# One gate product for both token halves in 32 stationary columns, in a kernel of attention and two expert layers

## The chip, the cores and the metric
One Trainium2 chip, one NeuronCore. The metric is the device time of one execution in microseconds (us), from the runs' own clock; beside it one execution was profiled, and its span runs from its first to its last instruction. Engines: TensorE (PE; its weight loads are PEld), VectorE (DVE), ScalarE (ACT), GpSimd (POOL) and SyncE (SP).

## The reference
Three layers, one behind the other: clustered attention (16 heads of 768 tokens, 64 wide), a routed expert layer (each of 1536 tokens goes to one of 8 experts) and a dense expert layer, in which the change lies. The last one is:

```python
def _moe2_ref(x, w_gate, w1, w2):          # x 1536x512, w_gate 512x8, w1 8x512x1024, w2 8x1024x512
    logits = x @ w_gate
    logits = logits - logits.max()
    P = np.exp(logits)
    for _ in range(8):
        P /= P.sum(1, keepdims=True) + 1e-09
        P /= P.sum(0, keepdims=True) + 1e-09
        P *= N / E
    out = np.zeros((N, D))
    for e in range(E):
        h = np.maximum(x @ w1[e], 0.0)
        out += P[:, e:e + 1] * (h @ w2[e])
    return out
```

## The kernel before
The program runs through attention (to about 310 us), the routed layer (19 tiles of 128 gathered tokens, to about 580 us), and the dense layer (to the end). Each engine has its own instruction list, written by hand, and semaphores join them; there is no planner. An engine works through its list in order, so a wait stops all that stands behind it.

**Numbers in two parts.** Products are made in fp32r with each operand split into a high part (a copy, `split_hi`, L877 to 879, ScalarE) and a low part (the operand less the high part, `split_lo`, L882 to 884, VectorE); a product of two operands is three: high x high, high x low, low x high. The profile gives the helper's line, L879 or L884, for all of them.

**The dense layer** splits tokens in halves (768 each, rows 1 and 2 of a 2x2 scheme), and the inner dimension in halves as well, and forms 7 products of sums of quarters where 8 would be plain ones. `XH[chunk]` and `XL[chunk]` hold, for one of two chunks of 384 tokens of each half (GN = 384), the transposed tokens' high and low parts as seven combinations, each of 2 slices of 128 rows: B11 (first half's tokens, first 256 inputs), B21 (first half's, last 256), B22 (second half's, last 256), T1 (second half's first 256 less first half's), and T2 to T4. The second half's first 256 inputs are so B11 + T1. A unit (L1369 on TensorE, L1635 on ScalarE, L2027 on VectorE) makes one 128-wide slice of two hidden halves for one chunk: seven `multiply` groups of 6 matmuls with 384 moving columns (L1321, L1323, L1324), and among them the six `second` groups of the unit before (L1344 to L1346, 6 matmuls with 512 moving columns each), whose sums VectorE adds to the output (L1959, L1962, L1968). Each expert has 8 units, so there are 64. Units alternate between the PSUM banks `ps_a[0]`, `ps_b[0]` and `ps_a[1]`, `ps_b[1]`; gate work of unit 1 uses the free ones of the other parity.

**The gate logits** are made in unit 1 of the first expert. `WG` (512x8 weights, 128 partitions x 4 x 8) is split in the last routed tile, by ScalarE (L1563) and VectorE (L1919), into `WGS` [128, 4, 16]: the high part in columns 0 to 7, the low part in 8 to 15 of each of 4 slices. `gate_logits(g, turn)` (L1287) makes a product with 16 stationary columns and 384 tokens moving into `ps_a[0]`, for g = 0 to 3: g % 2 is the chunk and g // 2 the token half. For the first half it takes B11 and B21 (4 slices), for the second B11, T1 and B22 (6 slices), each times the high and the low tokens (L1299). ScalarE copies the result to `LT` in SBUF (`read_logits_t`, L1604, L1608). `fold_logits` (L1303) then takes three 128-column pieces of `LT` as the stationary operand, with the small matrix `fold_e` (16x8, two identities on top of each other) moving (L1309), which transposes the logits to tokens on partitions and adds the high and low halves, into `ps_l` (bank `ps_b[0]`). Four turns follow each other: the next product waits until ScalarE has read the one before (`logits_t_out`), and ScalarE waits for the fold of the one before (`logits`). In the order of TensorE in unit 1: S2 stands for the `multiply` group of that name, and so on.

A11, S1, A12, second 0, gate(0), S2, fold(0), gate(2), second 1 and 2, S3, fold(2), gate(1), second 3 and 4, A22, fold(1), gate(3), second 5, S4, fold(3); then unit 2: A11, wait for `max_found`, S1.

VectorE copies the folded logits to `PROB` (L2081) at the end of its unit 1, behind the sum L2077 and the low part L1949 (which itself waits for ScalarE's relu L1676), and finds the maximum (L2083). Unit 2 of TensorE waits for that copy (L1388) ahead of its group S1, which overwrites the bank.

**The last routed tile** (L1913 on VectorE, L1559 on ScalarE, L1253 on TensorE) already sums token halves (`token_sums`: VectorE L1829 and L1831, GpSimd L2156 and L2159) and transposes and splits them for the dense layer (TensorE L1238; ScalarE `hi_parts`, VectorE `lo_parts`). On VectorE: `token_sums` 0 and 1, the gate's low part, the low part of the routed second weights, and the first `lo_parts`. On GpSimd ahead of the routed tiles (L2188 to L2200): two gathers (L2124), a memset of a zero tile (L2196), and the tile-row products (L2200). The constants, `fold_e` among them, are made by GpSimd at the very start (L94 to L117).

Of the kernel before, what the change touches and what calls it, by code (L numbers as in the profile page):

```python
# [72 lines left out]
def constants(nc, mem):  # L73
# [4 lines left out]
        "fold_e": mem.sbuf("fold_e", [2 * E, E]),  # L78
# [12 lines left out]
IDENT, ALL_MADE = 5, 9 + H - 1  # L91


def build_constants(pool, c, made):  # L94
# [20 lines left out]
    pool.wait_ge(made, 9)  # L115
# [757 lines left out]
GROUPS = NT // GT  # L873
# [31 lines left out]
def expert_layers(nc, sems, attn, c, X, L, w1, w2, xs, out_row, w_gate, dense_w1, dense_w2, out_dram, W1R, W1H, W1L,  # L905
                  w1_at, stationary_at, scratch_at, w1_loaded, x_stored):

    with ExitStack() as stack:
# [67 lines left out]
        WGS = mem.sbuf("w_gate_hi_lo", [P, DC, 2 * E], F32R)  # L976
# [31 lines left out]
        LT = mem.at("logits_t", [2 * E, GN], F32, stationary_at + 2 * STATIONARY * 4)  # L1008
# [26 lines left out]
        ps_l = ps_b[0][:, 0:NT * E].rearrange("p (t e) -> p t e", e=E)  # L1035
        ps_n = ps_m[:, GN:GN + NT * E].rearrange("p (t e) -> p t e", e=E)
# [27 lines left out]
        wg_loaded, wg_hi, wg_lo = mem.sem("wg_loaded"), mem.sem("wg_hi"), mem.sem("wg_lo")  # L1064
        x_t, x_hi, x_lo = mem.sem("x_t"), mem.sem("x_hi"), mem.sem("x_lo")
# [134 lines left out]
        def tensor(pe):  # L1200
# [86 lines left out]
            def gate_logits(g, turn):  # L1287

                if turn == 0:
                    pe.wait_ge(wg_lo, 1)  # L1290
                    pe.wait_ge(h_lo, 3)
                else:
                    pe.wait_ge(logits_t_out, turn)
                chunk, second_half = g % 2, g // 2
                terms = [(k, x) for k in range(DC) for x in (((B11, B21)[k // 2],) if not second_half else
                                                             ((B11, T1), (B22,))[k // 2])]
                for n, (k, x) in enumerate(terms):
                    for m, half_of in enumerate((XH, XL)):
                        mm = pe.matmul(ps_a[0][0:2 * E, 0:GN], WGS[:, k, :], half_of[chunk][:, x, k % 2, :],  # L1299
# [3 lines left out]
            def fold_logits(g, turn):  # L1303

                pe.wait_ge(logits_t_out, turn + 1)
                if turn == 0:
# [62 lines left out]
            def unit(e, q):  # L1369
# [25 lines left out]
                if first_expert and u == 1:  # L1395
                    gate_logits(0, 0)
# [903 lines left out]
```

## Time and profile before

| | before |
|---|---|
| median of 3 runs | 1614.45 us (1612.37 to 1615.25) |
| the profiled execution's own time | 1614.62 us |
| its span, first to last instruction | 1612.8 us |
| TensorE busy | 1578.4 us (98%), 8416 matmuls |
| VectorE busy | 1189.9 us (74%) |
| ScalarE busy | 771.0 us (48%) |
| GpSimd busy | 247.2 us (15%) |
| instructions | 27116 |
| mean granted TensorE clock | 0.994 |

How to read it: matmuls overlap in the records, so the distance from one start to the next is what a matmul costs in a row of them, and the duration beside it is longer. An idle time in brackets is that of the engine just before the instruction, with what released it. The granted clock of a window is a share of full speed.

### The profile page before, as it was taken

Reading aid. Unit: us, or ns where it says so; the run is one execution under the profiler, and the core shown is the slowest. Engines: PE = TensorE matmul, PEld = TensorE weight load, DVE = VectorE, ACT = ScalarE, POOL = GpSimd, SP = SyncE. Lnnn points to the kernel's source line nnn. Section 1 sums busy time; section 2 is a strip of 40 time slices with the busy share of each in tenths; the row PEclk is TensorE's granted clock in tenths of the full one; section 3 lists DMA queues with packets and bytes.
Section 4 is the critical chain, followed back from the end, with each engine's and each line's share of the span. In section 5 each row is a group of like instructions: output and inputs, shape, how many; then the busy total and the mean of one; then the engine's idle time right before and its main releaser. Section 6 shows DMA issues by size and latency. Waiting matters only on the chain.

```text
span 1612.8 us, 27116 instructions
## 1 busy us (share of the span) xinstructions
PE 1578.4 (98%) x8416; PEld 1397.6 (87%) x8416; DVE 1189.9 (74%) x2010; ACT 771.0 (48%) x1377; POOL 247.2 (15%) x314
## 2 busy tenths in 40 slices
PE   8999999899999989999999999999999999999998
PEld 7999999677777778898998989899898989989897
DVE  7999999999999974877665666656566665656664
ACT  5777779778888852322333233233323323222331
POOL 2111111213333350100010010001001000100102
PEclk8999999999999999999999999999999999999999
DMA  4223323354334310110010011001001100100002
GB/s 100 60 60 71 76 59 89 92 190 145 141 130 141 132 40 14 40 40 27 27 53 26 26 39 40 26 26 53 26 26 40 39 26 27 52 26 26 26 0 78
DMA packets 123699, 94.91 MB, mean 59 GB/s; under 512 B 66344, under 2 KB 101160, under 8 KB 123632
## 3 DMA queue, kind: packets, MB, share of 16 engines
q1 hardware_dynamic: 120848, 86.01, 17.7%
q0 software_dynamic: 2480, 8.13, 1.7%
q8 instruction: 21, 0.34, 0.1%
q14 instruction: 46, 0.38, 0.1%
q10 hardware_dynamic: 304, 0.05, 0.0%
HBM read 87.88 MB, written 6.29 MB: 58 GB/s over the span
## 4 chain that ended last, share of the span: by engine, by line
PE 88%; DVE 7%; issue 3%; ACT 2%; DMA 0%; DVEq 0%; SPq 0%; POOL 0%; ACTq 0%; POOLq 0%
PE moe_bank L1346 11%; PE moe_bank L1344 11%; PE moe_bank L1345 11%; PE moe_bank L1321 10%; PE moe_bank L1324 10%; PE moe_bank L1323 10%; PE attn_ps_out L441 2%; PE moe_bank L1267 2%; PE moe_bank L1269 2%; PE moe_bank L1268 2%; PE attn_ps_probs_t L422 2%; PE moe_bank L1280 2%; PE moe_bank L1282 2%; PE moe_bank L1281 2%; PE attn_ps_prep L347 1%
## 5 line engine op out<-in xcount | busy, mean ns | idle before, releaser
L1968 DVE SCALAR_TENSOR_TENSOR all_x<-moe_bank,all_x 128x512 f32<-128x512 f32 x336 | 251.3, 748 | 129.1 <-PE moe_bank L1346 126.4
L1321 PE MATMUL moe_bank<-moe_x_t_hi,all_w_hi 128*128 128x384 f32 x896 | 305.1, 341 | 3.0 <-DVE all_w_lo L884 2.9
L1324 PE MATMUL moe_bank<-moe_x_t_hi,all_w_lo 128*128 128x384 f32 x896 | 303.2, 338 | 0.0
L1323 PE MATMUL moe_bank<-moe_x_t_lo,all_w_hi 128*128 128x384 f32 x896 | 302.3, 337 | 0.0
L1344 PE MATMUL moe_bank<-moe_w_hi,moe_h_hi 128*128 128x512 f32 x768 | 301.1, 392 | 0.0
L1345 PE MATMUL moe_bank<-moe_w_lo,moe_h_hi 128*128 128x512 f32 x768 | 300.8, 392 | 0.0
L1346 PE MATMUL moe_bank<-moe_w_hi,moe_h_lo 128*128 128x512 f32 x672 | 265.0, 394 | 0.0
L1321 PEld LDWEIGHTS moe_bank<-moe_x_t_hi,all_w_hi 128*128 128x128 f32 x896 | 168.6, 188 | 14.0 <-issue 3.6
L1323 PEld LDWEIGHTS moe_bank<-moe_x_t_lo,all_w_hi 128*128 128x128 f32 x896 | 168.6, 188 | 11.3
L1324 PEld LDWEIGHTS moe_bank<-moe_x_t_hi,all_w_lo 128*128 128x128 f32 x896 | 168.5, 188 | 0.0
L1345 PEld LDWEIGHTS moe_bank<-moe_w_lo,moe_h_hi 128*128 128x128 f32 x768 | 144.2, 188 | 22.4
L1344 PEld LDWEIGHTS moe_bank<-moe_w_hi,moe_h_hi 128*128 128x128 f32 x768 | 144.4, 188 | 21.8
L2129 POOL TENSOR_TENSOR moe_w_sums<-moe_dense_w_raw 128x256 f32<-128x256 f32 x32 | 23.7, 740 | 853.0 <-DVE all_w_lo L884 853.0
L1346 PEld LDWEIGHTS moe_bank<-moe_w_hi,moe_h_lo 128*128 128x128 f32 x672 | 126.0, 188 | 28.6
L1676 ACT ACTIVATE moe_h_hi<-all_x 128x384 fp32r<-128x384 f32 x63 | 33.2, 526 | 169.4 <-DVE all_x L2077 169.4
L1648 ACT ACTIVATE moe_h_hi<-moe_p 128x384 fp32r<-128x384 f32 x63 | 33.2, 526 | 147.0 <-DVE moe_p L2036 147.0
L2036 DVE TENSOR_TENSOR moe_p<-moe_bank,moe_p 128x384 f32<-128x384 f32 x63 | 35.1, 557 | 90.7 <-PE moe_bank L1324 80.2
L884 DVE TENSOR_TENSOR moe_routed_w_lo<-moe_w_raw,moe_routed_w_hi 128x2048 fp32r<-128x2048 f32 x38 | 98.7, 2598 | 4.5 <-ACT moe_routed_w_hi L879 3.7
L637 DVE TENSOR_TENSOR attn_probs_t_lo<-attn_ps_probs_t,attn_probs_t_hi 128x384 fp32r<-128x384 f32 x192 | 97.1, 546 | 2.4 <-ACT attn_probs_t_hi L564 1.3
L1669 ACT ACTIVATE moe_h_hi<-moe_bank 128x384 fp32r<-128x384 f32 x63 | 31.0, 492 | 134.6 <-PE moe_bank L1324 134.6
L691 DVE CUSTOM_DVE_ANT_0 attn_scores<-attn_ps_scores,attn_mask 128x768 f32<-128x768 f32 x96 | 91.1, 949 | 2.6 <-issue 0.6
L558 ACT ACTIVATE attn_probs<-attn_scores,attn_row_max 128x768 f32<-128x768 f32 x96 | 91.3, 951 | 3.2 <-DVE attn_row_max L691 3.1
(325 smaller groups left out, 3065.7 us busy)
## 6 DMA issues: line engine op xcount, KB each, us to landing
all_w_raw<-in_moe_w SPq DMA_DIRECT2D x8, 2048.0 KB, 7.5
moe_w_raw<-in_moe_w SPq DMA_DIRECT2D x8, 2048.0 KB, 9.2
moe_dense_w_raw<-in_moe_w SPq DMA_DIRECT2D x64, 256.0 KB, 3.1
moe_dense_w_raw<-in_moe_w SPq DMA_DIRECT2D x32, 512.0 KB, 3.3
attn_q_raw<-in_q SPq DMA_DIRECT2D x32, 192.0 KB, 3.4
attn_k_raw<-in_k SPq DMA_DIRECT2D x32, 192.0 KB, 3.8
attn_v_raw<-in_v SPq DMA_DIRECT2D x16, 192.0 KB, 3.8
tokens<-all_x SPq DMA_DIRECT2D x32, 96.0 KB, 2.0
```

Source lines behind the costliest of these rows:

```text
L558: act.activation(PR[s % 2][:], SM[s % 2][:], ACT.Exp, bias=MX[s % 2][:], scale=-1.0, accum_out=SUM[:, s % 12:s % 12 + 1]).then_inc(exp_don ...
L637: return dve.tensor_tensor(out, src, hi.bitcast(F32), ALU.subtract)
L691: dve.tensor_tensor_reduce(out=SM[s % 2][:].rearrange("p (a k) -> p a k", a=2), in0=ps_s[s % 2][:, :, 0:3 * P], in1=MASK[s % 2][:].rearran ...
L884: return dve.tensor_tensor(out, src, hi.bitcast(F32), ALU.subtract)
L1321: pe.matmul(out, hi[:, s, k, :], XH[chunk][:, x, k, :], start=(start and k == 0), stop=False, skip_group_check=True)
L1323: pe.matmul(out, hi[:, s, k, :], XL[chunk][:, x, k, :], start=False, stop=False, skip_group_check=True)
L1324: mm = pe.matmul(out, lo[:, s, k, :], XH[chunk][:, x, k, :], start=False, stop=(stop and k == 1), skip_group_check=True)
L1344: pe.matmul(out, HH[h][hidden][:, rows], W2H[j][:, f, :], start=(f == 0), stop=False)
L1345: pe.matmul(out, HH[h][hidden][:, rows], W2L[j][:, f, :], start=False, stop=False)
L1346: mm = pe.matmul(out, HL[h][hidden][:, rows], W2H[j][:, f, :], start=False, stop=(f == 1))
L1968: dve.scalar_tensor_tensor(acc, y, PROB[:, row, bass.ds(at, 1)], acc, ALU.mult, ALU.add).then_inc(y_added, 1)
L2036: dve.tensor_tensor(CP1[:], m, CP1[:], ALU.add).then_inc(summed, 1)
```

## The change
The gate's weights stand in `WGS` [128, 4, 4, 16] now: for each slice four blocks of 16 columns, zeros in blocks 0 and 3, and the high and low parts in both block 1 and block 2. A product takes two neighbouring blocks as 32 stationary columns: blocks 1 and 2 add a slice to both token halves (B11, which both need), blocks 2 and 3 to the first 16 columns alone (B21), blocks 0 and 1 to the last 16 alone (T1, B22). So one group of 16 matmuls for a chunk makes the logits of both halves, and there are two turns in place of four. GpSimd clears `WGS` behind the first two gathers, ScalarE and VectorE split the weights twice. `fold_e` has 32 rows and 2 x 8 columns, and one fold writes both halves' logits of its three tiles. Gate(2) and fold(2) behind S2, and gate(3) and fold(3) are gone, so that unit 1 has: second 0, gate(0), S2, fold(0), second 1 and 2, S3, gate(1), second 3 and 4, A22, fold(1), second 5, S4.

```diff
-        "fold_e": mem.sbuf("fold_e", [2 * E, E]),
+        "fold_e": mem.sbuf("fold_e", [4 * E, 2, E]),
...
-    pool.tensor_tensor(c["fold_e"][:], c["ident"][0:2 * E, 0:E], c["ident"][0:2 * E, E:2 * E], ALU.add
-                       ).then_inc(made, 1)
+    for half in range(2):
+        at = 2 * E * half
+        pool.tensor_tensor(c["fold_e"][:, half, :], c["ident"][0:4 * E, at:at + E], c["ident"][0:4 * E, at + E:at + 2 * E],
+                           ALU.add).then_inc(made, 1)
...
-        WGS = mem.sbuf("w_gate_hi_lo", [P, DC, 2 * E], F32R)
+        WGS = mem.sbuf("w_gate_hi_lo", [P, DC, 4, 2 * E], F32R)
...
-        LT = mem.at("logits_t", [2 * E, GN], F32, stationary_at + 2 * STATIONARY * 4)
+        LT = mem.at("logits_t", [4 * E, GN], F32, stationary_at + 2 * STATIONARY * 4)
...
+        ps_l2 = ps_l.rearrange("p (c t) e -> p c t e", c=2)
...
-            def gate_logits(g, turn):
-
-                if turn == 0:
-                    pe.wait_ge(wg_lo, 1)
+            def gate_logits(chunk):
+
+                if chunk == 0:
+                    pe.wait_ge(wg_lo, 2)
                     pe.wait_ge(h_lo, 3)
                 else:
-                    pe.wait_ge(logits_t_out, turn)
-                chunk, second_half = g % 2, g // 2
-                terms = [(k, x) for k in range(DC) for x in (((B11, B21)[k // 2],) if not second_half else
-                                                             ((B11, T1), (B22,))[k // 2])]
-                for n, (k, x) in enumerate(terms):
+                    pe.wait_ge(logits_t_out, chunk)
+                terms = [(x, at, k) for x, at in ((B11, 1), (B21, 2), (T1, 0), (B22, 0)) for k in range(2)]
+                for n, (x, at, k) in enumerate(terms):
+                    w = WGS[:, 2 * (x in (B21, B22)) + k, at:at + 2, :].rearrange("p c w -> p (c w)")
                     for m, half_of in enumerate((XH, XL)):
-                        mm = pe.matmul(ps_a[0][0:2 * E, 0:GN], WGS[:, k, :], half_of[chunk][:, x, k % 2, :],
+                        mm = pe.matmul(ps_a[0][0:4 * E, 0:GN], w, half_of[chunk][:, x, k, :],
                                        start=(n == 0 and m == 0), stop=(n == len(terms) - 1 and m == 1))
                 mm.then_inc(logits_t, 1)
 
-            def fold_logits(g, turn):
+            def fold_logits(chunk):
...
-                    mm = pe.matmul(ps_l[:, g * GT + t, :], LT[:, t * P:(t + 1) * P], c["fold_e"][:],
-                                   start=True, stop=True)
+                    mm = pe.matmul(ps_l2[:, :, chunk * GT + t, :], LT[:, t * P:(t + 1) * P],
+                                   c["fold_e"][:].rearrange("p c e -> p (c e)"), start=True, stop=True)
...
-                split_hi(act, WGS[:, :, 0:E], WG[:]).then_inc(wg_hi, 1)
+                act.wait_ge(wg_zero, 1)
+                for copy in (1, 2):
+                    split_hi(act, WGS[:, :, copy, 0:E], WG[:]).then_inc(wg_hi, 1)
...
-                dve.wait_ge(wg_hi, 1)
-                split_lo(dve, WGS[:, :, E:2 * E], WG[:], WGS[:, :, 0:E]).then_inc(wg_lo, 1)
+                for copy in (1, 2):
+                    dve.wait_ge(wg_hi, copy)
+                    split_lo(dve, WGS[:, :, copy, E:2 * E], WG[:], WGS[:, :, copy, 0:E]).then_inc(wg_lo, 1)
...
-                    dve.wait_ge(logits, GROUPS)
+                    dve.wait_ge(logits, 2)
...
             gather(1)
+            pool.memset(WGS[:].bitcast(F32), 0.0).then_inc(wg_zero, 1)
```

## Rows read from the trace of the kernel before

**Rows 1.** The chain that ended last, share of the span by engine (the page)

```profile
PE 88%; DVE 7%; issue 3%; ACT 2%; DMA 0%; DVEq 0%; SPq 0%; POOL 0%; ACTq 0%; POOLq 0%
```

**Rows 2.** TensorE's waits, whole span: total us, times, longest us

```profile
PE moe_bank L1321 <- DVE all_w_lo L884: 2.9, 1, 2.9
PE moe_bank L1238 <- DVE moe_x_t_lo L884: 2.7, 4, 0.9
```

**Rows 3.** Windows: length, busy us of the engines, PE clock, DMA share, GB/s

```profile
560.00:564.00 4.00, 2.20 (x17) 1.89 (x16) 4.00 (x7) 2.33 (x6) 3.27 (x4) 1.00 0.17 65
...
596.00:598.00 2.00, 2.00 (x9) 2.00 (x8) 1.49 (x2) 0.95 (x2) 2.00 (x2) 0.53 0.00 0
...
640.00:680.00 40.00, 40.00 (x206) 36.09 (x205) 31.11 (x74) 14.10 (x26) 2.90 (x4) 1.00 0.09 27
```

**Rows 4.** Timeline of TensorE, 600 to 624 us: start us, us, what

```profile
603.17 0.34 PE L1324 MATMUL moe_bank<-moe_x_t_hi,all_w_lo 128*128 128x384 f32 x1
603.44 0.83 PE L1309 MATMUL moe_bank<-all_fold_e,moe_logits_t 16*128 16x8 f32 x6
604.20 0.35 PE L1299 MATMUL moe_bank<-moe_x_t_hi,moe_w_gate_hi_lo 128*16 128x384 f32 x1
...
621.39 0.34 PE L1324 MATMUL moe_bank<-moe_x_t_hi,all_w_lo 128*128 128x384 f32 x1
...
622.42 0.44 PE L1321 MATMUL moe_bank<-moe_x_t_hi,all_w_hi 128*128 128x384 f32 x1
...
623.39 0.34 PE L1324 MATMUL moe_bank<-moe_x_t_hi,all_w_lo 128*128 128x384 f32 x1
623.79 0.41 PE L1321 MATMUL moe_bank<-moe_x_t_hi,all_w_hi 128*128 128x384 f32 x1
```

**Rows 5.** The chain in order of time, 590 to 606 us: start us, us, what

```profile
597.13 0.32 PE moe_bank L1323
...
601.07 1.39 PE moe_bank L1299 x8
```

**Rows 6.** Instructions of L1299: ns min/median/max, first and last start us

```profile
L1299 PEld LDWEIGHTS moe_bank<-moe_x_t_hi,moe_w_gate_hi_lo x20: 93/94/95, 600.7 to 618.6; 128*16 128x16 f32 x20
L1299 PE MATMUL moe_bank<-moe_x_t_hi,moe_w_gate_hi_lo x20: 332/338/352, 600.9 to 618.8; 128*16 128x384 f32 x20
```

**Rows 7.** Costliest groups (the page): busy us, mean ns, idle before

```profile
L1321 PEld LDWEIGHTS moe_bank<-moe_x_t_hi,all_w_hi 128*128 128x128 f32 x896 | 168.6, 188 | 14.0 <-issue 3.6
```

**Rows 8.** Timeline of ScalarE

```profile
557.94 0.22 ACT L879 ACTIVATE moe_w_gate_hi_lo<-moe_w_gate_raw 128x32 fp32r<-128x32 f32 x1
...
602.50 0.48 ACT L1608 ACTIVATE moe_logits_t<-moe_bank 16x384 f32<-16x384 f32 x1 [1.66 <-PE moe_bank L1299]
...
622.36 0.53 ACT L1676 ACTIVATE moe_h_hi<-all_x 128x384 fp32r<-128x384 f32 x1 [2.56 <-DVE all_x L2077]
```

**Rows 9.** Timeline of VectorE

```profile
562.49 0.71 DVE L884 TENSOR_TENSOR moe_w_gate_hi_lo<-moe_w_gate_raw,moe_w_gate_hi_lo 128x32 fp32r<-128x32 f32 x1
563.12 2.28 DVE L884 TENSOR_TENSOR moe_routed_w_lo<-moe_w_raw,moe_routed_w_hi 128x2048 fp32r<-128x2048 f32 x1
...
621.77 0.56 DVE L2077 TENSOR_TENSOR all_x<-moe_bank,all_x 128x384 f32<-128x384 f32 x1 [0.36 <-PE moe_bank L1324]
622.92 0.56 DVE L1949 SCALAR_TENSOR_TENSOR moe_h_lo<-all_x,moe_h_hi 128x384 fp32r<-128x384 f32 x1 [0.59 <-ACT moe_h_hi L1676]
623.39 0.25 DVE L2081 COPY all_x<-moe_bank 128x96 f32<-128x96 f32 x1
```

**Rows 10.** Timeline of GpSimd

```profile
319.23 0.54 POOL L2196 MEMSET all_x<- 128x512 f32 x1
...
321.94 0.99 POOL L2124 DMA_INDIRECT moe_x_rows<-tokens,moe_token_of_item  x1 [0.64 <-PE moe_bank L1210]
...
562.25 0.91 POOL L2156 TENSOR_TENSOR moe_token_sums<-all_x,moe_token_sums 128x256 f32<-128x256 f32 x1
563.23 2.76 POOL L2159 TENSOR_TENSOR moe_token_sums<-all_x,moe_token_sums 128x256 f32<-128x256 f32 x1
```

More of the change, by code:

```diff
@@ L88, in constants @@
     return c, scratch_at, mem.sem("const_made")
-IDENT, ALL_MADE = 5, 9 + H - 1
+IDENT, ALL_MADE = 5, 10 + H - 1
 def build_constants(pool, c, made):
@@ L109, in build_constants @@
     pool.tensor_copy(c["identb"][:], c["ident"][:]).then_inc(made, 1)
-    pool.tensor_tensor(c["fold_e"][:], c["ident"][0:2 * E, 0:E], c["ident"][0:2 * E, E:2 * E], ALU.add
-                       ).then_inc(made, 1)
+    for half in range(2):
+        at = 2 * E * half
+        pool.tensor_tensor(c["fold_e"][:, half, :], c["ident"][0:4 * E, at:at + E], c["ident"][0:4 * E, at + E:at + 2 * E],
+                           ALU.add).then_inc(made, 1)
     pool.tensor_tensor(c["fold"][:, 0, 0:DH], c["ident"][:, 0:DH], c["ident"][:, DH:P], ALU.add).then_inc(made, 1)
-    pool.wait_ge(made, 9)
+    pool.wait_ge(made, 10)
     for h in range(1, H):
@@ L1064, in expert_layers @@
         wg_loaded, wg_hi, wg_lo = mem.sem("wg_loaded"), mem.sem("wg_hi"), mem.sem("wg_lo")
+        wg_zero = mem.sem("wg_zero")
         x_t, x_hi, x_lo = mem.sem("x_t"), mem.sem("x_hi"), mem.sem("x_lo")
@@ L1395, in unit @@
                 if first_expert and u == 1:
-                    gate_logits(0, 0)
+                    gate_logits(0)
                 if first_expert and u == 2:
@@ L1402, in unit @@
                 if first_expert and u == 1:
-                    fold_logits(0, 0)
-                    gate_logits(2, 1)
+                    fold_logits(0)
                 second(e, q - 1, 1)
@@ L1415, in unit @@
                 if first_expert and u == 1:
-                    fold_logits(2, 1)
-                    gate_logits(1, 2)
+                    gate_logits(1)
                 second(e, q - 1, 3)
@@ L1422, in unit @@
                 if first_expert and u == 1:
-                    fold_logits(1, 2)
-                    gate_logits(3, 3)
+                    fold_logits(1)
                 second(e, q - 1, 5)
@@ L1429, in unit @@
                 multiply(b, i, chunk, S4, B22, False, True).then_inc(cross, 1)
-                if first_expert and u == 1:
-                    fold_logits(3, 3)
             pe.wait_ge(found, ONE_HOT)
@@ L1607, in read_logits_t @@
                     act.wait_ge(logits, turn)
-                act.activation(LT[:], ps_a[0][0:2 * E, 0:GN], ACT.Copy).then_inc(logits_t_out, 1)
+                act.activation(LT[:], ps_a[0][0:4 * E, 0:GN], ACT.Copy).then_inc(logits_t_out, 1)
             def first_unit():
@@ L1653, in unit @@
                 act.activation(CU2, a, ACT.Copy).then_inc(copied, 1)
-                if logits_unit:
-                    read_logits_t(1)
                 if plain:
@@ L1666, in unit @@
                 if logits_unit:
-                    read_logits_t(2)
+                    read_logits_t(1)
                 act.wait_ge(chain, 4 * u + 4)
```

7 lines of the change are left out of this document (2 added, 5 removed).

## The prediction, made blind

> **What bounds the kernel now.** I read the chain that ended last first: TensorE holds most of it and VectorE a small part [rows 1]. Then TensorE's waits: the long ones all lie ahead of 600 us, behind VectorE's low parts [rows 2]. Then the windows: behind the changed stretch TensorE is busy without a gap (40.00 of 40 us) [rows 3], and the waits list none for it there, up to the end. So whatever is taken from TensorE in unit 1 comes off the end nearly whole, unless a wait takes its place; and what is added to VectorE ahead of 590 us, where TensorE waits for it, is paid too. Last I read the timelines of unit 1 (599.5 to 623.8 us), engine by engine.
>
> **Gate products (L1299).** Before there are 8 of them for each group of the first token half and 12 for each of the second, 2 x 8 + 2 x 12 = 40. After there are 16 for each chunk, 32 in all. One costs 1.39 / 8 = 0.174 us from start to start [rows 5]; its own 0.34 us [rows 6] overlaps the next. The eight that go are worth 8 x 0.174 = 1.39 us. Do the 32 wider ones cost more? The 16-column weight load takes 94 ns [rows 6], a 128-column one 188 ns [rows 7], and the 384-column products with 128 stationary columns also start about 0.174 us apart (603.17 stands in such a run) [rows 4]. The load is hidden at both widths, so nothing for 32 columns. The copy of the logits to SBUF, 16x384 in 0.48 us [rows 8], gets more partitions and no more columns: nothing.
>
> **Folds (L1309).** A fold stands between the product at 603.17 and the next one at 604.20 [rows 4]: 1.03 us for what would be 0.174, so it costs 0.86, plus 0.02 for a late start behind it. Four become two. The new ones have 16 moving columns instead of 8. A fold product holds (604.20 - 603.44) / 6 = 0.127 us, a product with 384 columns 0.174: 376 more columns cost 0.047 us, so eight more cost almost nothing. I take 0.05 us for both folds together, with ends 0 and 0.2.
>
> **What the order does with it.** The three folds ahead of unit 1's last product L1324 (621.39 [rows 4]) become two, and the fourth, behind it, goes too. So that product comes 1.39 + 0.88 = 2.27 us earlier, at 619.12. The fourth fold is different. Behind the last product stands a chain that does not shrink: VectorE's sum L2077 at 621.77 [rows 9], ScalarE's relu at 622.36 [rows 8], the low part at 622.92, and only then, as VectorE's queue is in order, the copy of the logits out of PSUM at 623.39 [rows 9]. The second product group of unit 2 waits for that copy (max_found) and starts at 623.79 [rows 4], 2.40 us behind 621.39. Before, TensorE filled this with the fold (622.42 - 621.39 - 0.174 = 0.86 us) and six products (to 623.39 + 0.174 = 623.56), and stood 0.23 us. After, it has the six products alone: ready at 619.12 + 0.174 + 6 x 0.174 = 620.34, released at 619.12 + 2.40 = 621.52. It stands 1.18 us, and **the fourth fold buys nothing**. Everything behind is relative to 623.79, which comes 2.27 us earlier.
>
> The other waits of unit 1 keep their cover. The first copy of the logits is now wanted behind gate(0) and the six products S2: eight products from 601.07 end at 602.46 in the chain [rows 5] and the copy begins at 602.50 [rows 8]; sixteen end at 603.85, so the copy runs from 603.9 to 604.4, and the fold wants it at 603.44 + 1.39 = 604.83. The second copy has two second-layer groups and six products (some 4 us) between the gate products and its fold, as before. VectorE's adds and ScalarE's copies wait for TensorE as before and shift with it; the weights of the next units are in place well before they are used.
>
> **What it adds ahead of that.** (a) VectorE's low part of the gate weights, now twice, in the last routed tile. The one there now starts at 562.49 and the next instruction at 563.12: 0.63 us for 32 elements a partition [rows 9], because GpSimd's L2156 runs from 562.25 for 0.91 us [rows 10]. TensorE waits for VectorE in this stretch (L1238 behind the low parts, 2.7 us in 4 waits [rows 2]), so this is paid. Undisturbed, a 128x96 copy takes 0.25 us [rows 9]. Bounds: -0.5 to +0.9 us. Above, the second part or the 563.12 split comes behind GpSimd's L2159 (which wants to start at 563.23 [rows 10]): nothing much for the part and 0.9, the length of L2156. Below, GpSimd would then be free up to 2 us sooner, since its L2159 took 2.76 us beside the split [rows 10], and later collide less. I take **+0.25**, the undisturbed row, since GpSimd's L2156 has just ended when the second part comes. By the Trainium skill, SBUF — State Buffer, section "SBUF: two separate sides", the ports that VectorE and GpSimd share are a lock held for a whole instruction, also for a VectorE operation with two SBUF inputs against a GpSimd operation that reads SBUF. By that rule the term is either the undisturbed price or the upper end, and nothing between; the 0.63 us and the 2.76 us agree with it.
> (b) ScalarE's second high part, 0.22 us like the first [rows 8]: ScalarE then waits for TensorE (its relu) and VectorE uses the parts 4 us later. Nothing; without that cover 0.22. (c) GpSimd's memset of the 256 elements a partition, between the gathers and the 319.23 memset, which takes 0.54 us for 512 [rows 10]: 0.27. The next gather at 321.94 stood 0.64 us waiting for TensorE [rows 10], so it is covered. The tile-row products move by 0.27 beside VectorE's norms: between -0.2 and +0.2, I take 0, as their number beside VectorE's work is the same. (d) A second fold matrix at the start, some 0.2 us of GpSimd: VectorE asks for the constants long after they are made. Nothing. (e) Longer buffers: 32 bytes and 768 bytes of addresses, no instruction.
>
> **Sum.** -1.39 - 0.88 + 0.05 + 0.25 = **-1.97 us**. The profiled execution took 1614.62 us (span 1612.8): 1612.65. The median shown is 1614.45, 0.17 below it, so **1612.5 us**. That is 0.12%. A measurement of this kernel tells some 0.2% (3.2 us) from no change, and its three runs already lie 2.9 us apart.
>
> **Rivals.** *Full gain.* The stall of 1.18 us doesn't appear, because the wait was not what held 623.79; then the start would come with TensorE's own work: 623.79 - 620.34 = 3.45 us, less 0.3: 1611.3. For it: the four folds and eight products really leave TensorE. Against: the wait stands in the code, and 0.23 us of it is already seen. With GpSimd ahead in (a) and less colliding later, the forecast also reaches there: 1611.8. Chance 0.15 for both.
> *TensorE's clock falls at the new stall.* In this kernel the clock stood at 0.53 in the window from 596 us [rows 3], the lower of its two levels for most of it, behind the 2.9 us wait [rows 2]; the products were 0.32 us apart instead of 0.174 [rows 5], ten of them: 1.5 us. The same at 621 us gives 1612.5 + 1.5 = 1614.0. Against: near 562 TensorE was busy for 2.20 of 4 us and the clock stayed at 1.00 [rows 3]. 0.07.
> *Slower: the second low part loses to GpSimd, and the clock falls with it.* Place: 563.12, decided by whether the low part of the routed weights starts behind L2159. Price 0.9 us of VectorE, passed to TensorE's waits, which are already dense there; with the clock down once (1.5 us) it is 0.9 - 0.25 + 1.5 = 2.15 above the forecast: 1614.7. It decides against the change when the two together pass 2.2 us. For it: TensorE stands 1.8 us of 4 there. Against: that alone left the clock up. 0.07; without the clock it is 1613.2 and inside the forecast. By the same section of the Trainium skill's page this end comes out whenever GpSimd's instruction starts first.
> *It doesn't do what it says*: 32 columns start at a slower pace, so that the 16 products take as long as 20: then 1.39 comes back, 1613.9. Against it: the 128-column products. 0.03.
>
> **Numbers.** Forecast 0.68, the rivals as above. The range takes the forecast with its bounds (-0.75 to +0.65, +0.2, +-0.2), the clock's case and a bit of the full gain: 1610.9 to 1614.8. Faster by over 0.2% needs 1611.2 or less: 0.16, from the full gain and the spread of the runs. Slower by over 0.2% would need three such mishaps: 0.03. Within 0.2%: 0.81.
>
> **What would show it.** In the changed profile: 32 gate products 0.174 us apart; two folds of some 0.8 us; from the first gate product (601.07 in the chain before) to the release of unit 2's second group 2.27 us less; a stall of about 1.2 us ahead of it, with VectorE's logits copy behind it; the two low parts near 562.5 and what GpSimd's L2159 does. It is wrong if that stall is missing, if the clock is low in it, or if TensorE's waits ahead of 600 us changed by more than 1 us.

## The result, and the profile after

| | before | after |
|---|---|---|
| median, runs side by side | 1613.66 us (1612.37 to 1615.25, 6 runs) | 1608.85 us (1606.64 to 1610.38, 6 runs) |
| ratio | | 0.9975, interval 0.9965 to 0.9984 |
| profiled execution, span | 1614.62, 1612.8 us | 1606.64, 1604.9 us |
| TensorE busy, matmuls | 1578.4 us, 8416 | 1571.1 us, 8396 |
| VectorE, ScalarE, GpSimd busy | 1189.9, 771.0, 247.2 us | 1190.3, 769.5, 248.4 us |
| instructions | 27116 | 27077 |

The changed kernel is **faster by 0.25%, some 4 us**, twice what was forecast, and outside the range given. 0.9975 of 1613.66 is 4.0 us less; the interval is 2.6 to 5.6 us. (The two medians of the table lie 4.8 us apart, inside that interval; all gains below are worked out from the ratios.)

The page of the changed kernel, its sums and the shares of the chain that ended last, beside [rows 1]:

```profile
PE 1571.1 (98%) x8396; PEld 1389.5 (87%) x8396; DVE 1190.3 (74%) x2011; ACT 769.5 (48%) x1376; POOL 248.4 (15%) x316
...
PE 88%; DVE 6%; issue 3%; ACT 2%; DMA 0%; DVEq 0%; ACTq 0%; POOL 0%; SPq 0%
```

The bound is the same: TensorE, with a little VectorE. The page alone says no more, so the time has to be looked for by stretches. I cut both timelines of TensorE at four marks that every version has. Times are us, read from starts of instructions:

| stretch | before | after | change |
|---|---|---|---|
| start to first routing product (attention) | 310.50 | 307.04 | -3.46 |
| to the first routed tile | 12.82 | 13.67 | +0.85 |
| to the first dense product (19 routed tiles) | 255.44 | 255.79 | +0.35 |
| to unit 2's second group (unit 0 and unit 1) | 45.03 | 41.87 | -3.16 |
| from there to the end of the dense layer | 989.00 | 986.44 | -2.56 |

The first row is not the change's: a second profiled execution of the very same changed kernel took 308.11 us there, and from the third head's scores (at 47 to 51 us) to the last scores every version took 248.0 to 248.3 us. What differs lies in the first 50 us, by where the clock's low level falls: from 12 to 28 us the mean granted clock is 0.68 in the trace of before and 0.90 in that of the changed kernel. Part of the fourth row is the clock too, and part of it a wait that nobody forecast (both below). The last row is the surprise: a stretch in which the change has no instruction is 2.56 us shorter. The second row needs care, as there too the clock differs: the window from 311.5 us of the changed kernel (columns as in [rows 3]) has it at the lower level throughout,

```profile
311.50:315.50 4.00, 4.00 (x14) 1.64 (x14) 3.76 (x16) 3.82 (x11) 2.08 (x2) 0.50 0.14 28
```

while before it is low only about 316 to 319 us.

**Unit 1 and the new stall, as forecast.** TensorE's timeline of the changed kernel, 597 to 619 us (start us, us, what), beside [rows 4]:

```profile
597.55 0.34 PE L1301 MATMUL moe_bank<-moe_x_t_hi,moe_w_gate_hi_lo 128*32 128x384 f32 x1
...
601.22 0.34 PE L1326 MATMUL moe_bank<-moe_x_t_hi,all_w_lo 128*128 128x384 f32 x1
601.50 0.84 PE L1311 MATMUL moe_bank<-all_fold_e,moe_logits_t 32*128 32x16 f32 x6
602.26 0.50 PE L1346 MATMUL moe_bank<-moe_w_hi,moe_h_hi 128*128 128x512 f32 x1
602.60 0.39 PE L1347 MATMUL moe_bank<-moe_w_lo,moe_h_hi 128*128 128x512 f32 x1
...
615.98 0.34 PE L1326 MATMUL moe_bank<-moe_x_t_hi,all_w_lo 128*128 128x384 f32 x1
616.15 0.34 PE L1323 MATMUL moe_bank<-moe_x_t_hi,all_w_hi 128*128 128x384 f32 x1
...
617.02 0.34 PE L1326 MATMUL moe_bank<-moe_x_t_hi,all_w_lo 128*128 128x384 f32 x1
618.37 0.42 PE L1323 MATMUL moe_bank<-moe_x_t_hi,all_w_hi 128*128 128x384 f32 x1 [1.01 <-DVE all_x L2077]
```

From the first gate product to unit 2's second group: 618.37 - 597.55 = 20.82 us. Before it was 623.79 [rows 4] less 600.91, where the timeline has the first gate product: 22.88. That is 2.06 us less. The last product of six could hand over at 617.02 + 0.17 = 617.19, the next group starts at 618.37: **TensorE stands 1.18 us**. (The bracket says 1.01, since it counts from the modelled end of the last record.) VectorE's timeline there, beside [rows 9]:

```profile
616.35 0.56 DVE L2073 TENSOR_TENSOR all_x<-moe_bank,all_x 128x384 f32<-128x384 f32 x1 [0.36 <-PE moe_bank L1326]
617.50 0.56 DVE L1945 SCALAR_TENSOR_TENSOR moe_h_lo<-all_x,moe_h_hi 128x384 fp32r<-128x384 f32 x1 [0.59 <-ACT moe_h_hi L1671]
617.97 0.25 DVE L2077 COPY all_x<-moe_bank 128x96 f32<-128x96 f32 x1
```

The chain sum, relu, low part, copy is the one of before, and TensorE starts 0.40 us behind the copy's start, as before (623.79 - 623.39). TensorE's waits in the changed kernel (total us, times, longest us), beside [rows 2]; the third is new and the only one behind 600 us:

```profile
PE moe_bank L1323 <- DVE all_w_lo L885: 2.9, 1, 2.9
PE moe_bank L1241 <- DVE moe_x_t_lo L885: 2.8, 4, 0.9
...
PE moe_bank L1323 <- DVE all_x L2077: 1.0, 1, 1.0
```

The windows about the stall (length, busy us of PE, PEld, DVE, ACT, POOL, PE clock, DMA share, GB/s), beside [rows 3]: the clock stays up in it.

```profile
616.00:618.00 2.00, 1.36 (x8) 1.04 (x6) 1.06 (x3) 0.95 (x2) 0.00 (x0) 1.00 0.25 97
618.00:620.00 2.00, 1.63 (x9) 1.66 (x10) 0.48 (x3) 0.00 (x0) 0.00 (x0) 1.00 0.03 8
```

The 32-column products: 16 of them hold 2.79 us in the chain, 0.174 each, the pace of [rows 5]. The line's own instructions (ns min/median/max, first and last start), beside [rows 6]; the weight load went from 94 to 108 ns and is hidden as before:

```profile
L1301 PEld LDWEIGHTS moe_bank<-moe_x_t_hi,moe_w_gate_hi_lo x16: 107/108/112, 597.3 to 608.4; 128*32 128x32 f32 x16
L1301 PE MATMUL moe_bank<-moe_x_t_hi,moe_w_gate_hi_lo x16: 332/336/341, 597.5 to 608.6; 128*32 128x384 f32 x16
```

**The two low parts.** VectorE, then GpSimd, in the last routed tile, beside [rows 9, 10]:

```profile
560.10 0.81 DVE L885 TENSOR_TENSOR moe_w_gate_hi_lo<-moe_w_gate_raw,moe_w_gate_hi_lo 128x32 fp32r<-128x32 f32 x2
560.84 2.28 DVE L885 TENSOR_TENSOR moe_routed_w_lo<-moe_w_raw,moe_routed_w_hi 128x2048 fp32r<-128x2048 f32 x1
```

```profile
560.84 2.86 POOL L2155 TENSOR_TENSOR moe_token_sums<-all_x,moe_token_sums 128x256 f32<-128x256 f32 x1
```

Both parts take 0.74 us from the first one's start to that of the 2048-element operation, one took 0.63: +0.11. VectorE's 2048-element part again comes first and GpSimd's sum stands behind it.

**What was not forecast, ahead of the first routed tile.** VectorE, then GpSimd, in the kernel before:

```profile
318.83 0.40 DVE L2094 TENSOR_SCALAR moe_sorted_tile<-moe_rounded_position 128x12 f32<-128x12 f32 x1
319.26 0.31 DVE L2095 TENSOR_TENSOR moe_tile_one_hot<-moe_tile_number,moe_sorted_tile 128x144 bf16<-128x144 f32 x1
```

```profile
318.05 1.18 POOL L2124 DMA_INDIRECT moe_x_rows<-tokens,moe_token_of_item  x1 [0.30 <-issue]
```

and in the changed one:

```profile
315.36 1.22 DVE L2090 TENSOR_SCALAR moe_sorted_tile<-moe_rounded_position 128x12 f32<-128x12 f32 x1
316.62 0.31 DVE L2091 TENSOR_TENSOR moe_tile_one_hot<-moe_tile_number,moe_sorted_tile 128x144 bf16<-128x144 f32 x1
```

```profile
314.59 1.17 POOL L2120 DMA_INDIRECT moe_x_rows<-tokens,moe_token_of_item  x1 [0.30 <-issue]
315.76 0.33 POOL L2190 MEMSET moe_w_gate_hi_lo<- 128x256 f32 x1
316.01 0.54 POOL L2193 MEMSET all_x<- 128x512 f32 x1
317.01 0.43 POOL L2197 TENSOR_TENSOR moe_tile_rows<-moe_tile_one_hot,moe_row_parts 128x144 bf16<-128x144 bf16 x1 [0.46 <-DVE moe_tile_one_hot L2091]
```

VectorE's small operation begins 0.8 us into the gather both times. Before, it ends with the gather (318.83 + 0.40 = 319.23, where [rows 10] has the one memset begin). After, it ends at 316.58, behind both memsets (316.55). GpSimd's products then stand 0.46 us for VectorE, which they had not done. What that is worth can't be read from this pair, as TensorE ran slowly here; it needs the experiments.

**What was not forecast either, behind the first dense product.** The first gate product comes 21.05 us behind the first dense product in the changed kernel (21.08 in its second trace). In a trace of the old instructions whose clock is up here too, that of the run with 768 bytes of padding below, it is 20.67. VectorE in that run:

```profile
594.75 0.56 DVE L1950 SCALAR_TENSOR_TENSOR moe_h_lo<-all_x,moe_h_hi 128x384 fp32r<-128x384 f32 x1 [0.59 <-ACT moe_h_hi L1633]
595.70 1.29 DVE L884 TENSOR_TENSOR moe_w_lo<-moe_dense_w_raw,moe_w_hi 128x1024 fp32r<-128x1024 f32 x1 [0.40 <-ACT moe_w_hi L879]
```

and in the changed kernel, VectorE, then TensorE:

```profile
593.40 0.93 DVE L1945 SCALAR_TENSOR_TENSOR moe_h_lo<-all_x,moe_h_hi 128x384 fp32r<-128x384 f32 x1 [0.59 <-ACT moe_h_hi L1631]
594.36 1.66 DVE L885 TENSOR_TENSOR moe_w_lo<-moe_dense_w_raw,moe_w_hi 128x1024 fp32r<-128x1024 f32 x1
```

```profile
596.07 0.50 PE L1346 MATMUL moe_bank<-moe_w_hi,moe_h_hi 128*128 128x512 f32 x1 [0.22 <-DVE moe_w_lo L885]
```

Both operations of VectorE take 0.37 us longer, and TensorE waits for the second, so **0.38 us are lost**. Beside them GpSimd forms the sums of the next weights, and starts these 0.15 us behind VectorE's `all_w_lo` (592.49 behind 592.34), where it starts 0.45 us behind it in the other trace. The six traces with the new instructions all have it so, at old addresses as at new ones, and with the memset early or late. Of the eight with the old instructions only one has it, that of the kernel before with one idle memset more on GpSimd (below). So one instruction more in GpSimd's list, over 270 us earlier, is enough; why GpSimd then starts sooner is not shown. The price appears in the two traces of the changed kernel alone: in the other five the clock is low here, and TensorE doesn't wait for `moe_w_lo`.

**The stretch with no change in it.** The first product of unit 0 of the second and of the last expert, on TensorE, before:

```profile
719.01 0.33 PE L1321 MATMUL moe_bank<-moe_x_t_hi,all_w_hi 128*128 128x384 f32 x1
...
1472.13 0.33 PE L1321 MATMUL moe_bank<-moe_x_t_hi,all_w_hi 128*128 128x384 f32 x1
```

and after:

```profile
713.60 0.34 PE L1323 MATMUL moe_bank<-moe_x_t_hi,all_w_hi 128*128 128x384 f32 x1
...
1464.48 0.34 PE L1323 MATMUL moe_bank<-moe_x_t_hi,all_w_hi 128*128 128x384 f32 x1
```

Six experts lie between: (1472.13 - 719.01) / 6 = **125.52 us each before, (1464.48 - 713.60) / 6 = 125.15 after**, and each of the six is the same to 0.01. The instructions are the same and the clock is full in both. The program's code there differs in nothing but the addresses of its buffers: `fold_e` grew by 32 bytes a partition and `WGS` by 768, and what is allocated behind each of them lies higher. The weights of the dense products (`all_w_hi`, `all_w_lo`) and the high parts of chunk 0's tokens are allocated ahead of both and do not move.

### The profile page after: what moved, and what is told of

It reads as the page before. It is cut to its first block, busy times and chain, and to the rows that moved or that the text cites. A ratio compares the mean times of both kernels' runs of the same rounds, so it can differ in the third digit from the quotient of the medians.

```text
span 1604.9 us, 27077 instructions
## 1 busy us (share of the span) xinstructions
PE 1571.1 (98%) x8396; PEld 1389.5 (87%) x8396; DVE 1190.3 (74%) x2011; ACT 769.5 (48%) x1376; POOL 248.4 (15%) x316
## 4 chain that ended last, share of the span: by engine, by line
PE 88%; DVE 6%; issue 3%; ACT 2%; DMA 0%; DVEq 0%; ACTq 0%; POOL 0%; SPq 0%
PE moe_bank L1346 11%; PE moe_bank L1348 11%; PE moe_bank L1347 11%; PE moe_bank L1323 10%; PE moe_bank L1326 10%; PE moe_bank L1325 10%; PE attn_ps_out L443 3%; PE attn_ps_probs_t L424 2%; PE moe_bank L1270 2%; PE moe_bank L1272 2%; PE moe_bank L1271 2%; PE moe_bank L1283 2%; PE moe_bank L1285 2%; PE moe_bank L1284 2%; PE attn_ps_prep L349 1%
## 5 line engine op out<-in xcount | busy, mean ns | idle before, releaser
L1323 PE MATMUL moe_bank<-moe_x_t_hi,all_w_hi 128*128 128x384 f32 x896 | 302.8, 338 | 3.9 <-DVE all_w_lo L885 2.9
L1323 PEld LDWEIGHTS moe_bank<-moe_x_t_hi,all_w_hi 128*128 128x128 f32 x896 | 168.4, 188 | 14.9 <-issue 4.5
```

What stands on the lines that cost most here:

```text
L1323: pe.matmul(out, hi[:, s, k, :], XH[chunk][:, x, k, :], start=(start and k == 0), stop=False, skip_group_check=True)
```

## The experiments

Two stories stood against each other for the 2.56 us: the buffers' new addresses, or something that the new gate work leaves behind (the order and phase in which unit 1 hands over to the loop). Beside them were to be tested the stall and the memset. All ratios below are to the kernel before, run on the same chip; an interval is given where there were rounds.

### The old instructions at the new addresses

```diff
         "fold_e": mem.sbuf("fold_e", [2 * E, E]),
+        "pad": mem.sbuf("pad", [P, 8]),
...
         WGS = mem.sbuf("w_gate_hi_lo", [P, DC, 2 * E], F32R)
+        mem.sbuf("pad", [P, 192])
```

> The kernel before with 32 bytes of padding behind fold_e and 768 bytes behind the gate weights: not one instruction is changed, but every buffer stands at the address it has in the changed kernel (most of the dense layer's at a multiple of 64 bytes in place of 32 past one). Theory A, the placement of the buffers gives the part that I did not forecast: an expert of the dense loop takes 125.15 us as in the changed kernel (125.52 before), and the time is some 2 to 2.5 us below the kernel before (ratio about 0.9986). Theory B, the excess is a matter of the single executions or of the removed instructions: 125.52 us an expert and a ratio of 1.000.

Measured: 1609.75 us against 1613.16, 0.9978 (0.9969 to 0.9987). An expert takes 125.15 us, and from unit 2's second group to the end it is 986.41 us, as in the changed kernel (986.44). To the first routed tile its profiled execution took 13.67 us, with no memset in it but with the clock low as long as in the changed kernel's: the 0.85 above is the clock's, and where the clock is low so long, TensorE covers what the memset costs. **More than half of what the change won comes with no change of an instruction.**

### The new instructions at the old addresses

`fold_e` and `WGS` are put in places of their own, and gaps of the old sizes keep everything else where it was. `WGS` lies in the end of a buffer that is in use until the squares are done, so its memset moves behind that wait.

```diff
-        "fold_e": mem.sbuf("fold_e", [4 * E, 2, E]),
+        "gap": mem.sbuf("gap", [P, E]),
+        "fold_e": mem.at("fold_e", [4 * E, 2, E], F32, 228544),
...
-        WGS = mem.sbuf("w_gate_hi_lo", [P, DC, 4, 2 * E], F32R)
+        mem.sbuf("gap", [P, 64])
+        WGS = mem.at("w_gate_hi_lo", [P, DC, 4, 2 * E], F32R, stationary_at - 1024)
...
-            pool.memset(WGS[:].bitcast(F32), 0.0).then_inc(wg_zero, 1)
             pool.wait_ge(squares, NT)
+            pool.memset(WGS[:].bitcast(F32), 0.0).then_inc(wg_zero, 1)
```

> The changed kernel with every buffer but the gate's two (fold_e and the gate weights, which lie in free places) at its address in the kernel before; GpSimd's memset of the gate weights stands behind the wait for the squares. Theory A: the dense loop is back at 125.52 us an expert and only my forecast of about -2.0 us is left of the gain (ratio 0.9988). Theory B: as the changed kernel, 0.9975 and 125.15 us.

Measured: 1611.06 us, 0.9990 (0.9981 to 1.0). An expert takes 125.52 us again. The new work alone shows here with the same clock as before: to unit 2's second group 42.99 us against 45.03, so **-2.04**; to the first routed tile 13.58 against 12.82, so **+0.76** (the memset, as VectorE's L2092 takes 1.22 us here too); the routed tiles 255.45 against 255.44. The sum is -1.3 us; the runs say -1.6 (0 to -3.1).

### The changed kernel again

> The changed kernel once more, beside the others on one chip. Both theories: a ratio of about 0.9975 (0.9965 to 0.9984), 125.15 us an expert. In unit 1 both say: unit 2's second group starts 20.82 us behind the first gate product (22.88 before, less 2.26 for it, and the spread of some 0.1), a stall of about 1.1 us ahead of it; where the clock is low differs from one execution to the next.

Measured: 1609.53 us, 0.9978 (0.9969 to 0.9987), on the chip of the two runs above; 125.15 us an expert. From the first gate product to unit 2's second group it takes 20.85 us, and TensorE stands 1.18 us. (The expectation's 2.26 us less is a slip: 22.88 to 20.82 are 2.06.) By time the kernel can't be told from the old instructions at the new addresses (1609.75): the new instructions' own -1.2 us is less than the 1.5 us to either side of each ratio. The traces tell it.

### The stall taken away

VectorE copies the folded logits ahead of the last second-layer sum instead of at the end of its unit.

```diff
                 low(u, hh, hl, Q21, a, 3)
+                if isinstance(u, int) and u == 1:
+                    dve.wait_ge(logits, 2)
+                    dve.tensor_copy(PROB, ps_l).then_inc(max_found, 1)
+                    dve.wait_ge(max_found, 1)
+                    dve.tensor_reduce(MXP[:], PROB, AX.XY, ALU.max).then_inc(max_found, 1)
                 add(e, q - 1, 5)
```

(The same five lines go from the end of the unit.)

> The changed kernel with VectorE's copy of the logits and the maximum of each partition ahead of the add of second group 5 of unit 1, in place of behind the last low part. If the chain sum, relu, low part, copy holds unit 2's second group, as I forecast, the stall of 1.0 to 1.2 us ahead of that group is gone and the time is 1.0 us below the changed kernel (ratio to before lower by 0.0006). If something else holds the group, the stall stays and nothing changes.

Measured: 1609.06 us, 0.9971 (0.9960 to 0.9981). The copy runs well ahead of its user, first VectorE, then TensorE around unit 2's second group:

```profile
617.72 0.25 DVE L2070 COPY all_x<-moe_bank 128x96 f32<-128x96 f32 x1
```

```profile
620.66 0.34 PE L1326 MATMUL moe_bank<-moe_x_t_hi,all_w_lo 128*128 128x384 f32 x1
620.83 0.34 PE L1323 MATMUL moe_bank<-moe_x_t_hi,all_w_hi 128*128 128x384 f32 x1
```

No gap is left. Unit 2 takes 16.25 us against 17.51, and the stretch from the first dense product to unit 2's second group 41.69 against 42.99 in the kernel with the new instructions at the old addresses, whose clock is low at the same place: 1.3 us. This is the fourth fold's 0.86 us and what TensorE stood there before, and it was behind VectorE's queue all along. The medians (0.5 us under the changed kernel's) don't resolve it.

### The memset moved

Behind the third gather, where GpSimd has waited for TensorE.

```diff
             gather(1)
-            pool.memset(WGS[:].bitcast(F32), 0.0).then_inc(wg_zero, 1)
...
                 gather(n + 2)
+                if n == 0:
+                    pool.memset(WGS[:].bitcast(F32), 0.0).then_inc(wg_zero, 1)
```

> The changed kernel with GpSimd's memset of the gate weights behind its third gather, where GpSimd has 20 us without work, in place of behind the second. Theory C: the memset, with the one behind it, holds VectorE's instruction TENSOR_SCALAR moe_sorted_tile (1.22 us in the profiles with it, 0.40 in the kernel before), and from the first routing product (moe_one_hot) to the first product of routed tile 0 it costs 0.8 us (13.58 with the clock low once near 315 us, 12.82 before). Then that instruction takes 0.40 us again and the kernel is 0.8 us faster than the changed one. Rival D: the gathers or the moved addresses do it; then 1.22 us and the longer stretch stay.

Measured: 1608.19 us against 1613.09, 0.9972 (0.9962 to 0.9982). VectorE, then GpSimd:

```profile
316.53 0.39 DVE L2090 TENSOR_SCALAR moe_sorted_tile<-moe_rounded_position 128x12 f32<-128x12 f32 x1
```

```profile
320.54 0.33 POOL L2201 MEMSET moe_w_gate_hi_lo<- 128x256 f32 x1
```

To the first routed tile it is 12.82 us again, so the 0.76 us is gone.

### Both moved

> The same, and VectorE's copy of the logits ahead of the add of second group 5. By the two theories both gains add: 0.8 and 1.0 us below the changed kernel, ratio to before about 0.9965. If they don't add, it is the clock that takes one back.

The two edits above in one kernel. Measured: **1607.29 us, 0.9965 (0.9951 to 0.9978)**, the lowest of all; 12.81 us to the first routed tile, unit 2 in 16.25. It beats the kernel before; that it beats the changed kernel rests on the trace, where it is 0.76 + 1.26 = 2.0 us shorter, as the intervals of the runs overlap.

### A memset alone, in the kernel before

```diff
+        IDLE = mem.sbuf("cleared_for_nothing", [P, 200])
...
             gather(1)
+            pool.memset(IDLE[:], 0.0)
```

> The kernel before with one more instruction: a memset of 200 elements a partition on GpSimd, into a buffer that nothing uses, behind the second gather. Theory C: VectorE's moe_sorted_tile takes about 1.1 to 1.2 us in place of 0.40, and routed tile 0 starts 0.7 to 0.8 us later against the first routing product (12.82 before). Rival D: 0.40 us and no shift. The dense loop stays at 125.52 us an expert.

One execution: 1614.3 us beside 1612.4 of the kernel before. VectorE, then GpSimd:

```profile
317.66 1.17 DVE L2095 TENSOR_SCALAR moe_sorted_tile<-moe_rounded_position 128x12 f32<-128x12 f32 x1
```

```profile
316.88 1.17 POOL L2125 DMA_INDIRECT moe_x_rows<-tokens,moe_token_of_item  x1 [0.30 <-issue]
318.06 0.28 POOL L2195 MEMSET moe_cleared_for_nothing<- 128x200 f32 x1
318.26 0.54 POOL L2198 MEMSET all_x<- 128x512 f32 x1
```

A memset that nobody reads is enough: 0.40 becomes 1.17 us, the end is that of the second memset (318.83 and 318.80), and the first routed tile comes 0.72 us later (13.54). An expert takes 125.52. That no wait stands between the gather and the new memset is not the reason either: in the kernel at the old addresses the wait for the squares stood between them, and VectorE's operation took 1.22 us all the same.

### Which bytes, and how many

Pads of other sizes behind `fold_e`, in the kernel before: 64 bytes (`[P, 16]`) and 96 (`[P, 24]`).

> The kernel before with 64 bytes of padding behind fold_e, no other edit: everything behind it moves by 64 bytes, so its place within 64 bytes stays. Theory A1, what counts is the place within 64 bytes: 125.52 us an expert in the dense loop, as before. Rival A2, any shift of the addresses changes the pace: another value.

> The kernel before with 96 bytes of padding behind fold_e: the place within 64 bytes is that of the changed kernel, the addresses are not. Theory A1: 125.15 us an expert. Rival A2: neither 125.15 nor 125.52.

Only the later part of the buffers by 32 bytes:

```diff
-        mem.fill("scratch_rest", scratch_at + 22 * KB + 512)
+        mem.fill("scratch_rest", scratch_at + 22 * KB + 512 + 32)
```

> The kernel before with 32 bytes of padding ahead of the second expert weights' raw buffer: the tokens' parts of chunk 1 and the low ones of chunk 0, the hidden parts of even units and both high parts of the second weights move to multiples of 64 bytes; the hidden parts of odd units, the first weights' raw buffer 1 and W2L of odd slices stay 32 past one, as does all of attention. If each operand counts by itself, an expert takes between 125.15 and 125.52 us, and attention keeps its time; if it is one buffer alone, it is 125.15 or 125.52.

And each pad of the first experiment by itself: 32 bytes behind `fold_e` (`[P, 8]`), and 768 behind `WGS` (`[P, 192]`).

> The kernel before with only the 32 bytes of padding behind fold_e (the first experiment of moved buffers had 768 bytes behind the gate weights as well, which move one raw buffer of the dense first weights alone). Theory A3, the operands of TensorE's products count: 125.15 us an expert with the 32 bytes alone. Rival: the raw buffer, which VectorE, ScalarE, GpSimd and the DMAs use, counts: 125.52.

> The kernel before with only the 768 bytes behind the gate weights. Theory A3: 125.52 us an expert, as before. Rival: 125.15. Something between in both runs would say that both count.

One execution each, so their times (1615.36, 1613.55, 1610.08, 1610.52 and 1612.36 us) settle nothing; the period of the loop does, as it repeats to 0.01 us within every trace:

| the kernel before, with | us an expert | from unit 2's second group to the end |
|---|---|---|
| nothing | 125.52 | 989.00 |
| 32 bytes behind `fold_e` | 125.15 | 986.42 |
| 64 bytes | 125.49 | 989.25 |
| 96 bytes | 125.41 | 988.48 |
| 32 bytes, later part only | 125.35 | 988.06 |
| 768 bytes behind `WGS` | 125.52 | 989.12 |

TensorE's timeline with the 32 bytes alone, at the two marks shown above for before:

```profile
717.47 0.34 PE L1322 MATMUL moe_bank<-moe_x_t_hi,all_w_hi 128*128 128x384 f32 x1
...
1468.35 0.34 PE L1322 MATMUL moe_bank<-moe_x_t_hi,all_w_hi 128*128 128x384 f32 x1
```

and with the 768 alone:

```profile
716.75 0.33 PE L1322 MATMUL moe_bank<-moe_x_t_hi,all_w_hi 128*128 128x384 f32 x1
...
1469.86 0.33 PE L1322 MATMUL moe_bank<-moe_x_t_hi,all_w_hi 128*128 128x384 f32 x1
```

(1468.35 - 717.47) / 6 = 125.15 and (1469.86 - 716.75) / 6 = 125.52. **The 32 bytes do it alone, and the 768 do nothing.** What lies only behind `WGS`, the raw dense weights among it, therefore doesn't count. It is not a matter of lying at a multiple of 64 bytes either, though nearly every buffer behind `fold_e` stood 32 past one before and stands on one after: by that, 96 bytes would be as good as 32. Both parts of the buffers count, since moving the later one alone gives some of it. Over the same six experts I summed the distances between starts by the pair of lines. 32 bytes take the step from a high x high product to the low x high one (before L1321 to L1323) from 176.8 to 174.4 ns, 672 of them: 1.6 us. Other pairs move by up to 0.9 us each, some one way and some the other, and bring the sum to 2.2. So single products of TensorE start some nanoseconds sooner or later. Which two addresses have to stand how to each other was not found, and stays open.

## Why the prediction was wrong

**Item (e), "Longer buffers: 32 bytes and 768 bytes of addresses, no instruction", is the step that failed.** It was put at nothing, without a reason. It measures -2.56 us behind unit 2's second group (-2.58 with the 32 bytes alone), and +0.22 in the routed tiles (255.66 against 255.44 us with the 32 bytes alone): -2.3 in all. The first reading, that what is taken from TensorE comes off the end whole, was right, and would have priced this term too, had anything been asked about it. No row of before could have given its size, but a term that no row prices needs bounds, and this one had none.

**(c), the memset "covered", failed in size.** Forecast 0 with ends of 0.2, measured +0.72 (alone) to +0.76 where the clock is low only for short, and nothing seen where it is low for long. The step looked at the work behind the memset on GpSimd's queue, the next gather and its 0.64 us of slack. It did not ask who runs beside it. The cover named was GpSimd's, and the one who paid was VectorE, whose result GpSimd's own next products want. The Trainium skill, SBUF — State Buffer, section "Who interferes with whom", says that a VectorE `tensor_scalar` can enter a mode that takes the port pair which it shares with GpSimd, and then one blocks the other for a whole instruction. The trace agrees in that 0.40 us became 1.22, to the end of GpSimd's memsets; that page's rule was used for the low parts, and should have been used here. It doesn't agree with the section's rule that whoever issues first gets the pair: VectorE's operation began 0.4 us ahead of the first memset and ended behind the second. No run here shows why one memset behind the gather lets VectorE in and two do not. The memset has a second price, the 0.38 us lost behind the first dense product where the clock is up. The prediction has no term for it.

**The gate products** are right: 32, 0.174 us apart, -1.39; the rival of slower 32-column products falls.

**The folds** are right: 0.76 us for a wide one (601.50 to 602.26), as narrow ones took (603.44 to 604.20), so the 0.05 for their width is 0. The copy of 32 rows of logits took 0.48 us as that of 16 had. The late start behind a fold was too small: I took 0.02, the row of a gate product; now a second-layer product of 512 columns follows both folds, and holds 0.34 us instead of 0.23 (602.26 to 602.60), so 0.2 in all. Unit 1 gave 2.06 (2.04 by the kernel at the old addresses) where 2.27 - 0.05 was forecast.

**"The fourth fold buys nothing"** is right, and so is the stall: 1.18 us forecast, 1.18 measured, with the copy of the logits behind the low part, and gone when the copy was moved. The rival without a stall falls. So does the one with the clock falling at it (1.00 in both windows).

**(a), the second low part**, came out at its undisturbed price or less: +0.11 on VectorE, and 0.01 to 0.13 in the routed tiles (the changed instructions at the old addresses less before; the changed kernel less the 32 bytes alone). The Trainium skill's rule (SBUF — State Buffer, section "SBUF: two separate sides"), by which it is one end or the other and nothing between, agrees: in all 14 traces the first part takes 0.71 to 0.72 us, beside GpSimd's sum, or 0.19, and the second part starts as if alone (0.10 us behind the first in the trace where both are undisturbed). The slower rival built on the other end falls. **(b) and (d)** cost nothing that a trace shows.

**TensorE's waits ahead of 600 us** hardly changed: [rows 2]'s 2.9 and 2.7 us are 2.9 and 2.8. (That they are all behind VectorE was read too narrowly: the list of before also has 4.5 us in 18 waits for ScalarE's `moe_h_rows` and 1.8 us for GpSimd's token sums, both the same after.) But behind the 2.9 us wait the clock, at 0.53 in the window at 596 us before [rows 3], stayed at 1.00 in this execution of the changed kernel. It is low there in the trace of the kernel with the 32 bytes alone (0.51) and not in the one with the 768, so it is not the change's. It is worth 1.5 us, by that last trace, which takes 43.55 us for the stretch where before took 45.03. So the table's -3.16 is -2.06 in unit 1, -1.5 of the clock, and +0.38 of the new wait for `moe_w_lo`.

**The sum again**, by traces: -2.56 + 0.22 (addresses) - 2.06 (unit 1) + 0.76 (memset) + 0.1 (low part) = **-3.5 us**, and -4.3 in an execution in which the low clock hides the memset; the wait for `moe_w_lo` takes 0.4 of the gain back where the clock is up at 595 us. The runs say -4.0 (-2.6 to -5.6), and -3.5 (-2.1 to -5.0) on the second occasion. The same terms give the others:

| version | by the traces' terms | by the runs, with interval |
|---|---|---|
| old instructions, new addresses | -2.3 | -3.5 (-2.1 to -5.0) |
| new instructions, old addresses | -1.3 | -1.6 (0 to -3.1) |
| changed, copy early | -4.8 | -4.7 (-3.1 to -6.5) |
| changed, memset late | -4.3 | -4.5 (-2.9 to -6.1) |
| changed, both | -5.6 | -5.6 (-3.5 to -7.9) |

By these terms the instructions alone would have made some 1612 us, and the run that has them at the old addresses had a median of 1611.06; both lie inside the forecast's range. So the mechanism in unit 1 was right, the memset was a miss that the +0.25 for (a) made good only in part, and the result left the range by a side effect. For the old instructions at the new addresses the traces' -2.3 and the runs' -3.5 lie 1.2 us apart, inside the interval; by the runs alone nearly the whole gain would be the addresses'. The chance of 0.16 for a gain over 0.2% was built on the full gain, which did not happen.

## What to carry to other kernels

A change of a buffer's size is a change of every address behind it, and in a kernel whose TensorE is busy for 98% of its time this can be worth as much as the change itself: give it bounds, and run the old instructions at the new addresses before a gain of some tenths of a percent is put down to the new ones. A piece of work put into a gap of one engine is free only if the engines that work beside it have nothing urgent at that time: here GpSimd had the gap and VectorE paid. And where work is taken from the bounding engine ahead of a wait, look at where the releasing instruction stands in its own queue: here moving a copy up was worth more than the fold that was removed.

## What was unexpected of the hardware

- Moving the buffers by 32 bytes took an expert's 125.52 us to 125.15, 64 bytes to 125.49, 96 to 125.41, with the same instructions at full clock. In the routed tiles the same 32 bytes cost 0.22 us, 64 bytes 0.8, and 96 bytes gave back 0.2 (one trace each).
- A GpSimd memset of 200 elements a partition (0.28 us) delayed a VectorE operation on 12 elements by 0.77 us, to the end of the memset behind it as well.
- With one memset more in GpSimd's list, its sums of weights over 270 us behind the memset start 0.30 us sooner, and two operations of VectorE beside them take 0.37 us longer each. All seven traces with a memset more show it, and none of the seven without.
- A weight load of 32 columns takes 108 ns where one of 16 takes 94 and one of 128 takes 188 [rows 6, 7]: some 80 ns of each don't depend on the columns (worked out from these three).
- In two profiled executions of the same changed kernel the low clock lies in different places: once none between 318 us and the last ten, once also at 323 and 565 us. At 595 us neither has it, and ten of the other twelve traces do. The profiled spans of that one program are 4.4 us apart (1604.9 and 1609.3), more than the whole change.
